# An expert's tile of 240 rows in two halves of 120, in place of 256 rows in two of 128

## The reference

```
logits = x @ w_gate                       # 8 experts
fresh  = argmax(logits)                   # expert of the token
e      = fresh if sigmoid(x @ w_local) < 0.5 or s == 0 else expert of the token before
h      = maximum(x @ w1[e], 0)            # 512 -> 1024
out    = softmax(logits)[e] * (h @ w2[e]) # 1024 -> 512
```

## Time and profile before

| | us |
|---|---|
| three runs | 473.89, 477.29, 477.82 |
| median | 477.29 |
| the profiled execution, device time | 476.8 |
| its span, first to last instruction | 475.1 |
| TensorE busy in the span | 429.8 (90%) |
| VectorE, ScalarE, GpSimd busy | 286.6, 211.7, 116.0 |

### The profile page before, as it was taken

The page is one execution under the profiler, slowest core; times in us unless marked ns, Lnnn a source line. Parts: engine busy times, 40 slices in busy tenths (PEclk is TensorE's granted clock), DMA queues, the critical chain, the costliest instruction groups (busy, mean ns, idle before and its releaser), DMA issues.

```text
span 475.1 us, 9670 instructions
## 1 busy us (share of the span) xinstructions
PE 429.8 (90%) x3108; PEld 385.3 (81%) x3109; DVE 286.6 (60%) x629; ACT 211.7 (45%) x415; POOL 116.0 (24%) x126
## 2 busy tenths in 40 slices
PE   3799999943999999999999999849989999999987
PEld 2788888833989898989898989649977779987775
DVE  3499999975555555555555656433687642477750
ACT  1123223251445454545464545414476644466653
POOL 0646465420110101010100000063049710015330
PEclk9999999985899999999999999959999999999999
DMA  7976657317768777676766684154220003220003
GB/s 235 311 255 209 209 176 237 139 68 281 257 215 294 257 253 248 244 251 241 256 230 221 221 285 157 38 146 127 69 65 2 1 24 112 61 71 0 0 0 132
DMA packets 32723, 78.37 MB, mean 165 GB/s; under 512 B 4032, under 2 KB 4160, under 8 KB 32704
## 3 DMA queue, kind: packets, MB, share of 16 engines
q1 hardware_dynamic: 25888, 58.21, 37.2%
q0 software_dynamic: 4512, 15.73, 9.7%
q10 hardware_dynamic: 2304, 4.20, 2.3%
HBM read 57.67 MB, written 17.30 MB: 158 GB/s over the span
## 4 chain that ended last, share of the span: by engine, by line
PE 76%; DVE 9%; issue 6%; DMA 5%; ACT 2%; SPq 1%; POOL 1%; DVEq 0%; ACTq 0%; POOLq 0%
PE bank L1189 7%; PE bank L1191 7%; PE bank L1190 7%; PE bank L1206 6%; PE bank L1204 6%; PE bank L1205 6%; PE bank L1308 5%; PE bank L1293 4%; PE bank L1275 3%; PE bank L1279 2%; PE bank L1251 2%; PE bank L1250 2%; PE bank L1249 2%; PE bank L1169 2%; DMA dec<-in_decay 2%
## 5 line engine op out<-in xcount | busy, mean ns | idle before, releaser
L1189 PE MATMUL bank<-xh,w1h 128*128 128x256 f32 x256 | 73.8, 288 | 0.9 <-DVE xl L905 0.9
L1191 PE MATMUL bank<-xh,w1l 128*128 128x256 f32 x256 | 73.6, 288 | 0.0
L1190 PE MATMUL bank<-xl,w1h 128*128 128x256 f32 x256 | 73.6, 288 | 0.0
L899 DVE TENSOR_TENSOR w2l<-raw,w2h 128x1024 fp32r<-128x1024 f32 x32 | 37.1, 1222 | 42.5 <-ACT w2h L583 42.5
L520 POOL TENSOR_SCALAR att<-att,stat,mixw 128x128 f32<-128x128 f32 (+5 forms) x48 | 34.0, 718 | 89.5 <-DVE stat L1038 89.5
L583 ACT ACTIVATE w2h<-raw 128x1024 fp32r<-128x1024 f32 x32 | 31.7, 1050 | 47.5 <-PE bank L1206 45.5
L1189 PEld LDWEIGHTS bank<-xh,w1h 128*128 128x128 f32 x256 | 50.5, 197 | 1.3 <-DVE xl L905 1.0
L1190 PEld LDWEIGHTS bank<-xl,w1h 128*128 128x128 f32 x256 | 50.4, 197 | 0.3
L1204 PE MATMUL bank<-w2h,hh 128*128 128x512 f32 x128 | 50.6, 395 | 0.0
L1191 PEld LDWEIGHTS bank<-xh,w1l 128*128 128x128 f32 x256 | 50.4, 197 | 0.0
L1206 PE MATMUL bank<-w2h,hl 128*128 128x512 f32 x128 | 49.9, 390 | 0.0
(11 more groups left out here) (158 smaller groups left out, 974.6 us busy)
## 6 DMA issues: line engine op xcount, KB each, us to landing
raw<-in_w SPq DMA_DIRECT2D x64, 512.0 KB, 5.9
xr<-tokens_by_expert POOLq DMA_DIRECT2D x8, 512.0 KB, 4.0
outputs_by_expert<-ysb ACTq DMA_DIRECT2D x16, 256.0 KB, 6.1
tokens_by_expert<-zero POOLq DMA_DIRECT2D x7, 512.0 KB, 6.2
q_in<-in_qT SPq DMA_DIRECT2D x12, 256.0 KB, 2.8
kz_in<-in_kT SPq DMA_DIRECT2D x24, 128.0 KB, 3.8
k_in<-in_kR SPq DMA_DIRECT2D x12, 256.0 KB, 3.8
v_in<-in_vR SPq DMA_DIRECT2D x12, 256.0 KB, 4.3
```

Source lines behind the costliest of these rows:

```text
L899: dve.tensor_tensor(part(low), raw[:, q, :], part(high).bitcast(F32), ALU.subtract).then_inc(w_lo, 1)
L1189: pe.matmul(to, w1h[:, dc, at], xh[:, dc, :], start=(dc == 0), stop=False)
L1190: pe.matmul(to, w1h[:, dc, at], xl[:, dc, :], start=False, stop=False)
L1191: last = pe.matmul(to, w1l[:, dc, at], xh[:, dc, :], start=False, stop=(dc == DC - 1))
```

## The change

`TILE` becomes 240, `TH` is fixed at 2, and a new constant `TR` = 120 is the number of rows in a half. `MAXT` (the most tiles that one expert can have) is rounded up, from 6 to 7. `MAX_TILES`, whose formula stands, goes from 13 to 14, and with it `CLEARED` from 2 to 3. The tiles `xr` and `ysb` keep 128 partitions but use 120; `xh`, `xl`, `hh`, `hl` shrink with `TILE`. Every access to a tile is narrowed to match. The number of instructions in a tile stays the same.

```diff
-TILE = 256
-TH = TILE // P
-MAXT = (B * S) // TILE
+TILE = 240
+TH = 2
+TR = TILE // TH
+MAXT = -(-(B * S) // TILE)
 MAX_TILES = (B * S + (E - 1) * (TILE - 1)) // TILE + 1
...
-                sp.dma_start(rows(ys, g * TILE, TILE).rearrange("(p a) n -> p (a n)", p=P), zero[:, :]).then_inc(ey_stored, 16)
+                sp.dma_start(rows(ys, g * TILE, TILE).rearrange("(p a) n -> p (a n)", p=TR), zero[0:TR, :]).then_inc(ey_stored, 16)
...
-            sp.dma_start(rows(xs, r, TILE).rearrange("(p a) n -> p (a n)", p=P), zero[:, :]).then_inc(first_padded, 16)
+            sp.dma_start(rows(xs, r, TILE).rearrange("(p a) n -> p (a n)", p=TR), zero[0:TR, :]).then_inc(first_padded, 16)
...
-            sp.dma_start(xr[:, :, :], rows(xs, 0, TILE).rearrange("(a p) n -> p a n", p=P)).then_inc(first_tile_in, 16)
+            sp.dma_start(xr[0:TR, :, :], rows(xs, 0, TILE).rearrange("(a p) n -> p a n", p=TR)).then_inc(first_tile_in, 16)
...
-                    act.activation(xh[:, 2 * j:2 * j + 2, :].rearrange("p a n -> p (a n)"), bank[:, 4 + j, :],
+                    act.activation(xh[:, 2 * j:2 * j + 2, :].rearrange("p a n -> p (a n)"), bank[:, 4 + j, 0:2 * TILE],
                                    ACT.Copy).then_inc(xh_ready, 1)
...
-                    act.activation(ysb[:, th, :], bank[:, 6 + th, :], ACT.Copy).then_inc(ey_ready, 1)
+                    act.activation(ysb[0:TR, th, :], bank[0:TR, 6 + th, :], ACT.Copy).then_inc(ey_ready, 1)
...
-                    act.dma_start(rows(ys, row, P), ysb[:, th, :]).then_inc(ey_stored, 16)
+                    act.dma_start(rows(ys, row, TR), ysb[0:TR, th, :]).then_inc(ey_stored, 16)
...
-                            last = pe.transpose(bank[:, 4 + j, c * TILE + th * P:c * TILE + (th + 1) * P],
-                                                xr[:, th, dc * P:(dc + 1) * P], ident)
+                            last = pe.transpose(bank[:, 4 + j, c * TILE + th * TR:c * TILE + (th + 1) * TR],
+                                                xr[0:TR, th, dc * P:(dc + 1) * P], ident[0:TR, 0:TR])
...
-                        at = slice(th * P, (th + 1) * P)
-                        to = bank[:, 6 + th, :]
+                        at = slice(th * TR, (th + 1) * TR)
+                        to = bank[0:TR, 6 + th, :]
```

More of the change, by code:

```diff
@@ L461, in _ @@
             for s in range(RING):
-                pool.dma_start(rows(ys, (E + s) * TILE, TILE).rearrange("(p a) n -> p (a n)", p=P), zero[:, :]).then_inc(scattered[s], 16)
+                pool.dma_start(rows(ys, (E + s) * TILE, TILE).rearrange("(p a) n -> p (a n)", p=TR), zero[0:TR, :]).then_inc(scattered[s], 16)
             with pool.Fori(1, NB // RING - 1) as k:
@@ L474, in pad @@
                 r = pool.value_load(pad_i[0:1, bass.ds(e, 1)], min_val=0, max_val=E * REGION - TILE)
-                pool.dma_start(rows(xs, r, TILE).rearrange("(p a) n -> p (a n)", p=P), zero[:, :]).then_inc(padded, 16)
+                pool.dma_start(rows(xs, r, TILE).rearrange("(p a) n -> p (a n)", p=TR), zero[0:TR, :]).then_inc(padded, 16)
             def load_tile(r):
-                pool.dma_start(xr[:, :, :], rows(xs, r, TILE).rearrange("(a p) n -> p a n", p=P)).then_inc(tile_in, 16)
+                pool.dma_start(xr[0:TR, :, :], rows(xs, r, TILE).rearrange("(a p) n -> p a n", p=TR)).then_inc(tile_in, 16)
             pool.wait_ge(pads_ready, 1)
@@ L598, in tile_out @@
                     act.wait_ge(ey_done, TH * (n - 1) + th + 2)
-                    act.activation(ysb[:, th, :], bank[:, 6 + th, :], ACT.Copy).then_inc(ey_ready, 1)
+                    act.activation(ysb[0:TR, th, :], bank[0:TR, 6 + th, :], ACT.Copy).then_inc(ey_ready, 1)
                     act.wait_ge(ey_ready, TH * (n - 1) + th + 2)
-                    row = nc.s_assert_within((n - 1) * TILE + th * P, 0, MAX_TILES * TILE - P,
+                    row = nc.s_assert_within((n - 1) * TILE + th * TR, 0, MAX_TILES * TILE - TR,
                                              skip_runtime_bounds_check_because=
                                              "there are at most MAX_TILES tiles, and n is at least one")
-                    act.dma_start(rows(ys, row, P), ysb[:, th, :]).then_inc(ey_stored, 16)
+                    act.dma_start(rows(ys, row, TR), ysb[0:TR, th, :]).then_inc(ey_stored, 16)
             act.wait_ge(route_ready, 1)
@@ L620, in expert @@
                         act.wait_ge(h_done, 4 * g + q + 1)
-                        act.activation(hh[:, 2 * q:2 * q + 2, :].rearrange("p a n -> p (a n)"), bank[:, q, :],
+                        act.activation(hh[:, 2 * q:2 * q + 2, :].rearrange("p a n -> p (a n)"), bank[:, q, 0:2 * TILE],
                                        ACT.Relu).then_inc(hh_ready, 1)
@@ L904, in tile_lo @@
                     dve.wait_ge(xh_ready, 2 * g + j + 1)
-                    dve.tensor_tensor(part(xl), bank[:, 4 + j, :], part(xh).bitcast(F32), ALU.subtract).then_inc(xl_ready, 1)
+                    dve.tensor_tensor(part(xl), bank[:, 4 + j, 0:2 * TILE], part(xh).bitcast(F32), ALU.subtract).then_inc(xl_ready, 1)
             for q in range(4):
@@ L930, in expert @@
                         dve.wait_ge(hh_ready, 4 * g + q + 1)
-                        dve.scalar_tensor_tensor(part(hl), bank[:, q, :], 0.0, part(hh).bitcast(F32),
+                        dve.scalar_tensor_tensor(part(hl), bank[:, q, 0:2 * TILE], 0.0, part(hh).bitcast(F32),
                                                  ALU.max, ALU.subtract).then_inc(hl_ready, 1)
```

## The result

| | before | changed |
|---|---|---|
| median of 20 runs, us | 475.27 | 478.17 |
| lowest, highest | 472.50, 478.39 | 472.94, 479.98 |
| profiled execution, device time | 476.8 | 473.3 |
| its span | 475.1 | 471.6 |

The changed kernel is slower: the ratio is 1.0058, with a 95% interval of 1.0037 to 1.0079. One run of 555.89 us, at a granted clock of 0.746, is a disturbed one; it counts in the median (477.85 without it), but is left out of the row of lowest and highest and of the ratio. The forecast was 472.7 us, a gain of 4.6.

A forecast was written before the change was run, and what follows sets the result against it. TensorE was taken to bound the kernel, with no waits in stage B. The terms -5.0 - 0.1 + 0.5 = -4.6 us, from the 477.29 us median, gave 472.7 us, range 469.3 to 477.7.

The forecast's parts named there:

- The first product: Stage B, lines 1189 to 1191: spacing falls from 119.9 to 113.2 ns; 740 matmuls save 5.0 us.
- weights: Stage B's first expert matmuls: the weight load sets the spacing, so nothing is gained; 477.7 us, chance 0.22.
- floor: Stage B's first expert matmuls: overhead vanishes once the stream is shorter than the load, 109 ns; 469.6 us, chance 0.05.
- fp32r under 256 columns: Stage B's first expert matmuls: the narrower stream runs at two cycles a column; 546 us, chance 0.05.
- Eight tiles: Stage B: at most 232 tokens an expert keep 8 tiles; a ninth would make 495 us, chance 0.03.
- The third clear: Stage A: one more SyncE DMA of 480 KB ahead of the fourth block's loads; 0 to 1.7 us, +0.5 taken.
- The DMAs: Pads, tile loads and stores carry fewer bytes from 120 rows; -0.5 to +0.5 us, 0 taken.
- The second product: Stage B: halves of 120 stationary columns beside an unchanged 512-column stream; 0 us, 0.5 us at most.
- Cover: Stage B: weights keep up with experts of 22.7 us; otherwise a shortfall of 0.6 us an expert at most.
- ScalarE, VectorE: PSUM reads at most 6% or 37 ns shorter, covered by TensorE except at the first tile; -0.1 us.
- route: A few VectorE operations on one partition treat 56 elements in place of 48; under 0.1 us.
- first rival: Stage B: the weight load, not the streamed columns, sets the spacing, so nothing is gained; 477.7 us, chance 0.22.

The follow-up runs named there:

- full version: Kernel before with 240-token tiles in 256-row buffers and loads, clears from 128 partitions, one clear moved behind the first tile's load: 470.26 us, ratio 0.9898.

## Why the prediction was wrong

**The first product: right.** 113.2 ns were forecast, 112.2 measured; 5.0 us forecast, 5.1 measured alone (by the ratio's interval, 3.0 to 6.6). At the lower clock they gave nothing, as expected. TensorE's timeline of the first expert, in the version with the narrowed stream alone:

```profile
118.19 0.41 PE L1190 MATMUL bank<-xh,w1h 128*128 128x240 f32 x1
...
119.89 0.39 PE L1192 MATMUL bank<-xh,w1l 128*128 128x240 f32 x1
```

That is 1.70 us for 8 steps, 213 ns, as with 256 columns in the earlier trace rows, though 240 columns alone are 200 ns at 1.2 GHz. So something that does not follow the streamed columns sets the spacing there; the weight load, the prediction's reason, fits but was not tried by itself. Three rivals fall at the full clock: no spacing of 120 (weights), none of 109 (floor), none above 200 (fp32r under 256 columns keeps one column a cycle: 240 are 100 ns, plus 12). The Trainium skill ("TensorE: Matmul & The Clock Gate", "Back-to-back issue gap") gives N/2.4 + 2.5 for a single matmul in isolation, 102.5 ns here; the trace's 112.2 disagrees, and its step from 256 to 240 columns, 7.7 ns, is close to 16/2.4 plus 1.

**Eight tiles: right.** 256 matmuls a line.

**The third clear: the step that failed, by its size.** The prediction named every link: v late, GpSimd's clears late behind the decay, the row copy waiting for them. It then took +0.5 from 0 to 1.7 us, "since most has slack". The ceiling was wrong. 1.7 us was the clear's transfer time, but the price is set at the end of the chain, where TensorE stops and in some runs the clock falls. The prediction looked for slack at the fourth block's matmuls, where more than 5 us are to spare (its operand is ready at 28.44, its use at 34.92); the slack that counts is the 1.2 us at `xT`. Alone the clear cost 5.1 us in the medians, with one group of runs untouched; in the changed kernel its removal gave 2.8.

**The DMAs: the other step that failed.** "I take 0, the middle of -0.5 and +0.5." The pad and the first load came out at +0.4 and +0.8 us, above the upper end together, and the last store, left unpriced, at +0.3 (the pad's part varies, as shown above). The largest part was not in the list at all: the clears of stage A go from 120 partitions as well, and that alone costs 2.75 us. The rule of the Trainium skill ("DMA: Bandwidth & Descriptors", "Why a DMA increments its semaphore by 16 and not by 1"), 15 engines with 8 rows each, would by an estimate leave a 120-row transfer as long as a 128-row one. The rows disagree: 2.39 against 2.06. Nor does it fit 112 rows, which divide by 16 and still took 2.28. No run here shows how many engines a transfer used.

**The second product: wrong.** Costed at 0, with 0.5 us as the upper end. 8 phases times 0.23 us are 1.8 us. The cover was named (the load lies beside the stream), and the overhead of the stream was assumed not to depend on the stationary width. With only the width changed it does, 234 ns for 227. How much of the changed kernel's 0.23 us a phase belongs to it is open, since the version with 128 columns kept most of that.

**Cover, ScalarE, VectorE, route: right**, as far as the profile shows. TensorE has no wait in stage B after the first tile.

**The account.** Changed kernel minus full version, 478.17 - 470.26, is 7.9 us (7.6 without the disturbed run). Clears from 120 partitions 2.75 (medians), early third clear 0.9 (medians, unsure, net of what its late place costs), second product 1.8 (phases), pad, first load and last store 0.4 (10.78 in the changed kernel's chain, 10.34 in the full version's): 5.9. Against the kernel before, whose three transfers take 9.34, the last item is 1.4. The other 2.0 are not settled. It may be that two delays of one chain cost more together once the slack is gone, but that was not separated, and the row copy's waits, one profile each, scatter too much to show it (with three early clears 4.6 to 8.3 us).

**The numbers.** The forecast started from a median of three runs, 477.29; twenty runs give 475.27. The same -4.6 us from there would be 470.7, so the start, too high by 2.0 us, brought the forecast nearer to the 478.17 by luck. The change itself was missed by 7.5 us: -4.6 forecast, +2.9 measured. The range's upper end, 477.7, fell 0.5 us short even so. It was the time of the first rival, with no gain in the first product, and not of a case in which several small costs on one chain eat the gain.

## What to carry to other kernels

Cost a shrunken tile by where it goes: the streamed columns pay at once, but the same constant also sets partitions of transfers, stationary width and the number of housekeeping copies, and each needs its own price. Here it paid to narrow the compute and to leave buffers and most transfers at 128 partitions. A wait behind which a queue stands has slack and then a cliff: price a delay by what TensorE loses past the slack, clock included, not by the length of the transfer.

## What the runs showed of the hardware

- Stores from 120 or 112 partitions took longer than from 128, with fewer bytes: 2.39 to 2.42 and 2.27 to 2.28 us against 2.06 to 2.09. Three clears issued together, of the same bytes, took 4.1, 8.0 and 9.1 us to landing from 120 partitions and 3.1, 4.7 and 6.3 from 128.
- 120 stationary columns (and output partitions) in place of 128 slowed a 512-column fp32r stream from 227 to 234 ns a matmul, in the version that changes only them.
- fp32r with 240 streamed columns took 112.2 ns a matmul at 2.4 GHz, 100 ns of columns and 12 on top; at 1.2 GHz it took 213, as 256 columns do.
- In a stop of TensorE of 3.7 us in stage A the granted clock fell to 1.2 GHz and stayed there for 6.8 us; the changed kernel's profiles, which lost 1.05 and 1.3 us in the same window, kept 2.4 GHz there.
